# Routing steps on VectorE, the load order of the first expert, and where PE reads its loop bounds, in an attention and mixture-of-experts kernel

## The reference

```python
# q, k, v: (2, 8, 576, 64); x below: 1152 tokens x 512
scores = where(mask, (q @ k.T) / 8, -1e9)
x = softmax(scores) @ v
# first mixture: E = 8, F = 1024
logits = x @ w_gate + modality_bias[modality_id]
e_idx = argmax(logits); gate_w = softmax(logits)[e_idx]
out[mask_e] = gate_w * (relu(x[mask_e] @ w1[e]) @ w2[e])    # for each e
# second mixture: 4 experts, p = normalised domain_probs
out2 = sum_e p[:, e] * (relu(out @ w1[e]) @ w2[e])
```

## Time and profile before

| | us |
|---|---|
| median of 3 runs | 639.79 |
| lowest, highest | 636.93, 640.26 |
| the profiled execution, its own time | 640.29 |
| its span, first to last instruction | 638.5 |
| PE busy in the span | 609.7 (95%) |
| DVE busy | 359.8 (56%) |
| ACT busy | 207.2 (32%) |
| POOL busy | 300.1 (47%) |
| mean granted PE clock | 0.978 of full |

### The profile page before, as it was taken

One profiled execution on the slowest core, in us unless ns is written; L12 is line 12 of the kernel. 1 busy time (PEld: TensorE's weight loads), 2 busy tenths in 40 slices (PEclk: granted clock), 3 DMA queues, 4 the chain that ended last, 5 costly groups with the idle time before them and its releaser, 6 DMA issues.

```text
span 638.5 us, 10555 instructions
## 1 busy us (share of the span) xinstructions
PE 609.7 (95%) x3604; PEld 531.9 (83%) x3605; DVE 359.8 (56%) x735; ACT 207.2 (32%) x528; POOL 300.1 (47%) x278
## 2 busy tenths in 40 slices
PE   5998899899999999999999999999999999999996
PEld 4887767687666788998998998998998998998894
DVE  5879576225787532368546546545545545545554
ACT  3866242224667522222311311321321221231230
POOL 6535220163000000944999676467568458547005
PEclk9999588899999999999999999999999999999999
DMA  9914524833887010200212220120111120110003
GB/s 230 237 9 166 223 91 149 296 100 70 285 291 257 18 33 16 67 1 1 67 66 67 67 66 16 52 67 28 37 66 33 33 66 33 33 66 0 0 0 148
DMA packets 27091, 56.68 MB, mean 89 GB/s; under 512 B 6840, under 2 KB 9528, under 8 KB 27064
## 3 DMA queue, kind: packets, MB, share of 16 engines
q1 hardware_dynamic: 18632, 31.93, 16.0%
q0 software_dynamic: 6848, 21.52, 10.1%
q10 hardware_dynamic: 1584, 2.88, 1.8%
HBM read 48.97 MB, written 7.36 MB: 88 GB/s over the span
## 4 chain that ended last, share of the span: by engine, by line
PE 82%; DMA 6%; issue 4%; DVE 4%; POOL 2%; ACT 2%; SPq 0%; DVEq 0%; ACTq 0%; POOLq 0%
PE bank L1470 29%; PE bank L1441 28%; PE bank L1364 8%; PE bank L1376 6%; PE bank L1289 3%; DMA x_by_expert<-zero_row 2%; DMA w_raw<-in_moe_w 1%; POOL out L573 1%; DVE w_lo L868 1%; PE bank L1354 1%; PE bank L1326 1%; PE bank L1299 1%; PE bank L1255 1%; PE bank L1284 1%; DMA kT<-in_kT 1%
## 5 line engine op out<-in xcount | busy, mean ns | idle before, releaser
L1161 DVE SCALAR_TENSOR_TENSOR acc<-bank,meta_s,acc 128x512 f32<-128x512 f32 x135 | 100.8, 749 | 62.2 <-PE bank L1470 62.1
L1470 PE MATMUL bank<-u_hi,h_hi 128*128 128x512 f32 x288 | 112.3, 390 | 0.0
L1470 PE MATMUL bank<-u_lo,h_hi 128*128 128x512 f32 x288 | 112.1, 389 | 0.0
L1470 PE MATMUL bank<-u_hi,h_lo 128*128 128x512 f32 x288 | 112.0, 389 | 0.0
L1208 DVE SCALAR_TENSOR_TENSOR h_lo<-bank,h_hi 128x288 fp32r<-128x288 f32 x112 | 50.9, 455 | 44.7 <-ACT h_hi L735 22.9
L1441 PE MATMUL bank<-x2T_hi,u_hi 128*128 128x288 f32 x232 | 68.4, 295 | 0.0
L1441 PE MATMUL bank<-x2T_lo,u_hi 128*128 128x288 f32 x232 | 68.4, 295 | 0.0
L1441 PE MATMUL bank<-x2T_hi,u_lo 128*128 128x288 f32 x232 | 68.3, 295 | 0.0
L1441 PE MATMUL bank<-t_hi,u_hi 128*128 128x288 f32 x224 | 66.2, 295 | 0.0
L1441 PE MATMUL bank<-t_lo,u_hi 128*128 128x288 f32 x224 | 66.0, 295 | 0.0
L1441 PE MATMUL bank<-t_hi,u_lo 128*128 128x288 f32 x224 | 65.9, 294 | 0.0
(11 more groups left out here) (226 smaller groups left out, 1284.4 us busy)
## 6 DMA issues: line engine op xcount, KB each, us to landing
w_raw<-in_moe_w SPq DMA_DIRECT2D x10, 2048.0 KB
u_raw<-in_moe_w POOLq DMA_DIRECT2D x16, 512.0 KB, 3.7
u_raw<-in_moe_w POOLq DMA_DIRECT2D x16, 256.0 KB, 3.1
u_raw<-in_moe_w POOLq DMA_DIRECT2D x32, 128.0 KB, 2.8
x_tile<-x_by_expert ACTq DMA_DIRECT2D x11, 256.0 KB, 2.7
x_by_expert<-zero_row SPq DMA_DIRECT2D x10, 256.0 KB, 2.2
qT<-in_qT SPq DMA_DIRECT2D x4, 576.0 KB, 8.4
kT<-in_kT SPq DMA_DIRECT2D x8, 288.0 KB, 10.1
```

The costliest lines, as they stand in the source:

```text
L1161: w.scalar_tensor_tensor(out=acc[:, t, :], in0=bank[Z_BANK[i]][:], scalar=meta_s[:, t, bass.ds(e + 1, 1)], in1=acc[:, t, :], op0=ALU.mult, ...
L1470: last = t_.matmul(bank[Z_BANK[i]][:], lhs[:, c, ts], rhs[page][:, c, :], start=c == 0 and k == 0, stop=c == 1 and k == 2)
```

## The change

Four things are done.

1. On DVE, `keep_ranks` reads the ranks in PSUM and multiplies them with the one-hot rows, and no multiplication is left in `find_slots`. `e_rows` is added by PE instead, with a matmul of `ones` on a new constant `e_part` (`e_rows` / 128, whose sum over 128 partitions is `e_rows`). The copies and sums of `x_first` and `slot` become steps with one tensor input.
2. `put_in_order` and `find_bases` leave attention; the first goes to the head of `count_tiles`, the second to the head of `place_tiles`, and `is_e0` behind `fill_known`.
3. SP loads w2 in two halves behind the load of the first rows; ACT waits for the first half (`w2_early`) and later for the second.
4. PE reads `n_runs` and `n_tiles` in the second tile, ahead of its last four matmuls.

```diff
@@ SP
             sp.wait_ge(x_first_known, 3)
-            sp.dma_start(w2_raw[:].unsqueeze(1),
-                         w2[bass.ds(expert, 1)].rearrange("e (c p) d -> p e c d", p=P)).then_inc(w2_in, 16)
...
             sp.dma_start(x_tile[:], xb[bass.ds(x0, P), :]).then_inc(xt_in, 16)
+            for half, done in ((0, w2_early), (1, w2_in)):
+                f = slice(FH * half, FH * (half + 1))
+                sp.dma_start(w2_raw[:, f].unsqueeze(1),
+                             w2[bass.ds(expert, 1), HALF * half:HALF * (half + 1)].rearrange("e (c p) d -> p e c d", p=P))\
+                  .then_inc(done, 16)
@@ ACT
-            act.wait_ge(w2_in, 16)
+            act.wait_ge(w2_early, 16)
             cut_w2(0)
             cut_w2(1)
             keep_h(0, 0)
+            act.wait_ge(w2_in, 16)
             cut_w2(2)
@@ DVE
             def keep_ranks(tiles, src):
-                w.tensor_tensor(rank_e[:, tiles, :], src.rearrange("p (t e) -> p t e", e=E),
-                                e_rows[:].unsqueeze(1).to_broadcast([P, n, E]), ALU.add).then_inc(vstep, 1)
+                w.tensor_tensor(rank_e[:, tiles, :], src.rearrange("p (t e) -> p t e", e=E), onehot[:, tiles, :],
+                                ALU.mult).then_inc(vstep, 1)
...
             def find_slots(tiles):
-                step(w.tensor_tensor(rank_e[:, tiles, :], rank_e[:, tiles, :], onehot[:, tiles, :], ALU.mult))
                 step(w.reduce_sum(slot_f[:, tiles], rank_e[:, tiles, :], axis=AX.X))
-                w.tensor_copy(slot[:, tiles], slot_f[:, tiles]).then_inc(slot_ready, 1)
+                w.tensor_scalar(slot[:, tiles], slot_f[:, tiles], 0.0, None, ALU.add).then_inc(slot_ready, 1)
...
-                w.tensor_copy(x_first[:, 0:1], choice[:, 2:3]).then_inc(x_first_known, 1)
-                w.tensor_tensor(x_first[:, 3:4], choice[:, 2:3], choice[:, 0:1], ALU.add).then_inc(x_first_known, 1)
-                w.tensor_tensor(x_first[:, 1:2], choice[:, 2:3], choice[:, 3:4], ALU.add).then_inc(x_first_known, 1)
+                w.tensor_scalar(x_first[:, 0:1], choice[:, 2:3], 0.0, None, ALU.add).then_inc(x_first_known, 1)
+                w.tensor_scalar(x_first[:, 3:4], choice[:, 2:3], choice[:, 0:1], None, ALU.add).then_inc(x_first_known, 1)
+                w.tensor_scalar(x_first[:, 1:2], choice[:, 2:3], choice[:, 3:4], None, ALU.add).then_inc(x_first_known, 1)
...
-                if m == CHOSEN_AT + 3:
-                    put_in_order()
-                if m == CHOSEN_AT + 4:
-                    find_bases()
...
             def count_tiles():
+                put_in_order()
...
             def place_tiles():
+                find_bases()
@@ PE
             def rank_group(t0, t1, where):
+                last = t_.matmul(where.rearrange("p (t e) -> p t e", e=E), ones[:],
+                                 e_part[:].unsqueeze(1).to_broadcast([P, t1 - t0, E]),
+                                 start=False, stop=True, skip_group_check=True)
...
                 h_w2(r, second, ht_hi, w2_lo)
+                known = bounds and bounds()
                 pe.wait_ge(ht_kept, j * NHALF + 2)
                 h_w2(r, second, ht_lo, w2_hi).then_inc(y_done, 1)
...
-            whole_tile(1, 0)
-
-            pe.wait_ge(table_ready, 1)
-            n_runs = pe.value_load(table[0:1, 4, 0:1], min_val=1, max_val=E)
-            n_tiles = pe.value_load(table[0:1, 4, 1:2], min_val=EARLY + 1, max_val=MAXT)
+            n_runs, n_tiles = whole_tile(1, 0, loop_bounds)
```

More of the change, by code:

```diff
@@ L179, in moe_chain @@
         e_rows = sb("e_rows", [P, E])
+        e_part = sb("e_part", [P, E], BF16)
         rank_e = sb("rank_e", [P, NT, E])
@@ L314, in moe_chain @@
         scattered = sem("scattered")
-        w1_in, w2_in = sem("w1_in"), sem("w2_in")
+        w1_in, w2_in, w2_early = sem("w1_in"), sem("w2_in"), sem("w2_early")
         xt_in, xt_flipped, xt_hi_kept, xt_kept = sem("xt_in"), sem("xt_flipped"), sem("xt_hi_kept"), sem("xt_kept")
@@ L452, in _ @@
             g.iota(e_rows[:], pattern=[[ROWS, E]], base=0, channel_multiplier=0,
+                   allow_small_or_imprecise_dtypes=True).then_inc(consts, 1)
+            g.iota(e_part[:], pattern=[[ROWS // P, E]], base=0, channel_multiplier=0,
                    allow_small_or_imprecise_dtypes=True).then_inc(consts, 1)
@@ L969, in _ @@
             w.tensor_tensor(fill_at[:], n_tok[:], e_rows[:], ALU.add).then_inc(fill_known, 1)
+            step(w.tensor_scalar(is_e0[:], e_down[:], choice[:, 1:2], None, ALU.is_equal))
             dve.wait_ge(fill_known, 1)
@@ L1258, in rank_group @@
             def rank_group(t0, t1, where):
-                last = t_.matmul(where, before[:], onehot[:, t0:t1, :].rearrange("p t e -> p (t e)"), start=True, stop=True)
+                t_.matmul(where, before[:], onehot[:, t0:t1, :].rearrange("p t e -> p (t e)"), start=True, stop=True)
+                last = t_.matmul(where.rearrange("p (t e) -> p t e", e=E), ones[:],
+                                 e_part[:].unsqueeze(1).to_broadcast([P, t1 - t0, E]),
+                                 start=False, stop=True, skip_group_check=True)
                 for t in range(t1 - 1):
@@ L1379, in h_w2, with loop_bounds, second_layer @@
                 return last
-            def second_layer(j, r):
+            def loop_bounds():
+                pe.wait_ge(table_ready, 1)
+                return (pe.value_load(table[0:1, 4, 0:1], min_val=1, max_val=E),
+                        pe.value_load(table[0:1, 4, 1:2], min_val=EARLY + 1, max_val=MAXT))
+            def second_layer(j, r, bounds=None):
                 first, second = range(FH), range(FH, FCH)
@@ L1391, in second_layer, with whole_tile @@
                 h_w2(r, second, ht_hi, w2_lo)
+                known = bounds and bounds()
                 pe.wait_ge(ht_kept, j * NHALF + 2)
                 h_w2(r, second, ht_lo, w2_hi).then_inc(y_done, 1)
-            def whole_tile(j, r):
+                return known
+            def whole_tile(j, r, bounds=None):
                 pe.wait_ge(xt_kept, j + 1)
@@ L1402, in whole_tile @@
                 flip_x(j + 1)
-                second_layer(j, r)
+                return second_layer(j, r, bounds)
             flip_x(0)
```

7 lines of the change are left out of this document (3 added, 4 removed).

## The result

The changed kernel takes **630.35 us** (median of 4 runs, 629.76 to 631.74) beside 638.46 us for the kernel before (median of 4 runs, 636.93 to 640.26; 639.79 was the median of three of them). The ratio is 0.9875, with a 95% interval of 0.9838 to 0.9912. The forecast started from the profiled execution, 640.29. Of the 5.0 us between 635.3 and 630.35 the sum is short by 3.55 (8.55 measured from profile to profile, 5.0 summed), and 1.4 are that the profiled execution after, 631.74, is the slowest of its four.

The account below looks back on a forecast made before the run. From 254.4 us on, matmuls bind the kernel (PE busy 378 of 384 us), so all gain lies ahead of 118 us. Terms -0.8 - 1.8 - 0.2 - 0.4 - 1.8 = -5.0 from 640.29 gave 635.3 us, range 632.5 to 638.9.

Parts of the forecast that it names:

- A: Attention's tail, DVE at 55 to 64 us: shorter and moved routing steps bring POOL's scatters and PE's last transposes earlier, -0.8.
- R3: Rival, chance 0.08: the new scalar steps on DVE lock like L848, so A is only -0.5; 635.6 us.
- B: First tile: with w2 behind the first rows, PE's whole wait ahead of the transposes of `x_tile` goes, -1.8.
- R4: Rival, chance 0.07, 0.05 of it slower: w2 comes too late for ACT's wait `w2_in`; 642.2 us.
- C: Third group: one DVE step fewer between PE's ranks and the scatter, second tile's rows earlier, -0.2; moved `is_e0` costs 0.
- D: Loop's entry: PE's bound loads, moved ahead of the second tile's last four matmuls, start the loop earlier, -0.4.
- E: Loop's entry: PE's clock doesn't fall behind two shorter pauses, the 12 matmuls take 2.7 to 2.9 us, -1.8.
- R1: Rival, chance 0.28: the clock falls at the loop's entry all the same; 637.1 us, or 638.1 with D at +0.6.
- R2: Rival, chance 0.12: fewer PE waits keep the clock at 2.4 GHz longer in attention's tail, -1.7; 633.6 us.

Follow-up runs that it names:

- the run with w2 alone: The kernel before with only w2 loaded in halves behind the first rows: 637.76 us, ratio 0.9956.
- w2 as before: The changed kernel with w2 loaded in one piece in its old place, ahead of the rows of zeros: 636.43 us, ratio 0.993.
- `is_e0` early: The changed kernel with only the step making `is_e0` moved ahead of the last `w_lo` of w1 on DVE: 634.69 us, ratio 0.9928.

## Why the prediction was too small

**What bounds the kernel** held for this pair: the second mixture's 384 us stand unchanged, and each microsecond won ahead of 118 us came through.

**A** (-0.8, measured -0.98 on PE). The first scatter starts at 59.05, which is 58.37 less the offset; 58.3 was written. This term holds in the second pair of profiles too: counted from `choice<-count_a`, POOL's third scatter comes at 10.93 and 10.92 in before and 10.05 and 10.04 in after, 0.88 earlier. No short step at 55 to 64 us is above 0.28, so R3 is refuted: one input and a scalar of a single element doesn't lock. The steps that answer to the earlier trace rows:

```profile
56.21 0.20 DVE L848 TENSOR_SCALAR x_first<-choice 128x1 int32<-128x1 f32 x1
56.33 0.20 DVE L849 TENSOR_SCALAR x_first<-choice 128x1 int32<-128x1 f32 x1
...
58.47 0.28 DVE L831 TENSOR_SCALAR slot<-slot_f 128x3 uint32<-128x3 f32 x1
```

**B** (-1.8, measured -1.83 for the wait itself, -2.04 from the last transposes of `xT` to those of `x_tile`). SP's timeline, which answers to the earlier trace rows:

```profile
55.48 0.39 SPq L368 DMA_DIRECT2D w_raw<-in_moe_w  x1
57.85 0.38 SPq L374 DMA_DIRECT2D x_by_expert<-zero_row  x1
68.48 0.36 SPq L377 DMA_DIRECT2D x_tile<-x_by_expert  x1
68.94 0.95 SPq L380 DMA_DIRECT2D w_raw<-in_moe_w  x2
```

The load of the first rows goes out 3.6 us earlier. ACT cuts w2 at 78.01 (81.26 in the earlier trace rows) behind its own work, so R4 never had its condition. The run with w2 alone fits: its trace has no wait there, and its median, a noisy one, is 2.8 lower.

**C** (-0.2) is the step that failed. Its gain for group 3 is there (0.22, one DVE step less), but the sentence "`is_e0` now comes behind `fill_known`, which no one awaits urgently" priced the moved step at 0. I looked for who waits for that step, and not at what stands behind it on DVE and whom that shuts out. It is worth 1.35 us of PE's wait and, through the clock, 1.56 more: 2.9 us in the profiled pair, 2.6 and 3.6 us by the medians of the two runs that move or add nothing but it. In the second pair of profiles it is larger: 1.47 of wait and 2.47 in the matmuls. With 2.9 in the sum, -5.0 is -7.9, against the 8.5 measured. The trace of before showed that something stood there: scatters of 1.97 and 1.43 where 1.0 to 1.2 is the rule, and a mark of 1.31 on PE at 95.87, which the prediction never named. That the moved step fell on the good side of a gap of 0.15 us (1.09 against 1.24) was luck.

**D** (-0.4, measured -0.42). The loads answer to the earlier trace rows, with the columns of there:

```profile
L1390 PEldq TENSOR_LOAD <-table x1: 490/490/490, 104.6 to 104.6; - x1
L1391 PEldq TENSOR_LOAD <-table x1: 312/312/312, 105.5 to 105.5; - x1
```

The table was ready at 104.53, and the first load went at once: the sequencer no longer stood at a matmul. With the bounds behind the tile as before it stood there again: the table was ready at 105.88, and the first load went at 107.1, with the last four matmuls (107.13), so the rule of the Trainium skill that I set against the row (Advanced Engine Details and Errata, "Sequencer Loop") would have put it 1.2 us earlier, and the measurement decides against that reading. The pauses are 0.94 and 0.80 where 1.0 and 0.9 were written. In the run with `find_bases` earlier the first of them is 0.15.

**E** (-1.8, measured -1.60, 3.01 for 4.61). 2.7 to 2.9 was written for the twelve matmuls; behind a pause they take 3.0 at the full clock. That the clock rides out a pause in two pieces was a guess without a row behind it. It held in the profile of after and in four others with two pauses of 0.80 to 0.88 us, and in two where the first is only 0.15 and 0.19; it failed in two (w2 as before, 0.82 and 0.88; `is_e0` early, 0.85 and 0.86), which is R1. So the sizes of the pauses don't tell the two kinds apart, and what does is open. Where the pause was one of 2.3 us, the clock fell in all five profiles.

**R2** (the clock kept longer in the tail) came true in part in the profiled pair: it fell 0.9 us later, for which 0.86 us stand in the account. Its rise came earlier too, at 78.64 instead of 84.59, but for the routing of group 3 PE then waited 0.95 for DVE (80.59, in the rows of PE), so that this brought nothing. The second pair doesn't repeat it: the change run again fell at 62.01 and the kernel before run again at 64.34. So these 0.86 us are luck of the pair, as far as four profiles show.

The upper end of the range is 0.4 off by its own terms: R1's 637.1, half of A (0.4) and D at +0.6 instead of -0.4 (1.0) make 638.5, and 638.9 was written. Nothing hangs on it.

A sum then: -0.98 (A), -0.86 (R2), -2.04 (B), -0.22 (C), -2.91 (the race and the clock behind it), -0.42 (D), -1.60 (E), and +0.68 for the later start, is -8.35, of 8.46 at the loop's first tile; the rest are gaps between these places. The parts are not independent: undone one by one they cost 4.3 (w2), 4.9 (bounds), 1.9 (order) and 2.3 us (routing) against the 632.08, 13.4 together for a gain of 8.9. In three of the four the profile has a fall of the clock at the second tile or at the loop's entry that the change doesn't have. A pause at one place can bring a fall that another part had kept away; how much of the overlap this is, against executions of one kernel that spread over 3 to 8 us, isn't shown.

What stays open: why the clock sometimes keeps up through pauses at which it falls in other runs. No run varied only that. What sets the length of the first stretch of low clock in an execution is as open. No version here beats the change by more than a measurement can tell.

## What to carry to other kernels

Where an engine's instruction takes longer in some places than in others (a scatter of 1.97 beside 0.96), look up what the neighbouring engine does in those microseconds, before costing any edit that shifts either by a tenth: such a place is a switch and not a slope, and a step that nobody waits for can throw it. Put the short steps that nobody waits for between a release for POOL and the long two-input steps of DVE, so that POOL's work goes first. And cost a pause of PE with the clock that may fall behind it; here a wait of about 1 us was worth 2.6 to 3.7 in the medians.

## What the hardware showed beyond that

- GpSimd's issue of an indirect DMA that comes while DVE's `w_lo` runs lasts until some 0.85 us behind the end of that step (89.11 for 88.26 in before): 1.96 and 1.43 us, for 0.96 alone. Between two such steps of DVE in one go it gets in only if it already stands there. `w_lo` isn't lengthened by a scatter that came first.
- Behind a wait of 0.87 to 1.47 us and a second one of 1.40 the granted clock fell in five profiles and stayed in one (only w2, 1.14 and 1.40). With the 1.40 alone it stayed in all of eight.
- The same program's executions differ by up to 8 us, and the granted clock goes with it: the run without the first part took 628.05 us at a mean of 0.995 and 635.98 at 0.982.
